# MLP and experts on one core: POOL rounds and subtracts the expert weights alone, in a ring of five raw and three high buffers, and splits the next group's x; ranks one chunk later

## The reference, cut to what matters

```python
# attention: B=4, H=8, S=576, D=64, causal window of 64
x = attn_out.transpose(0, 2, 1, 3).reshape(2304, 512)
# MLP: w_in 512x2048, w_out 2048x512
h = x @ w_in
x2 = (h * sigmoid(1.702 * h)) @ w_out
# mixture of 8 experts: w1 512x1024, w2 1024x512, two experts per token
noisy = x2 @ w_gate + log1p(exp(x2 @ w_noise)) * noise
top2 = the two largest of 8;  w = softmax over the two
out[token] = sum over both of w * (relu(x2[token] @ w1[e]) @ w2[e])
```

## Time and profile before

| what | value |
|---|---|
| median of 3 runs (lowest, highest) | 1072.35 us (1068.4, 1073.0) |
| the profiled execution's own time | 1068.85 us |
| its span, first to last instruction | 1067.2 us |
| mean granted TensorE clock | 0.974 of full |
| busy: TensorE, weight loads | 991.4, 849.1 us |
| busy: VectorE, ScalarE, POOL | 568.7, 509.5, 385.9 us |
| DMA | 225.22 MB, 211 GB/s over the span |

### The profile page before, as it was taken

How to read it: one execution, slowest core, us unless ns; L and a number is a source line. 1 busy time by engine, 2 the same in 40 slices (tenths; PEclk the granted TensorE clock), 3 DMA queues, 4 the chain that set the end, 5 groups by cost and what they waited for, 6 DMA issues and landing times.

```text
span 1067.2 us, 19690 instructions
## 1 busy us (share of the span) xinstructions
PE 991.4 (93%) x5424; PEld 849.1 (80%) x5425; DVE 568.7 (53%) x1340; ACT 509.5 (48%) x1216; POOL 385.9 (36%) x416
## 2 busy tenths in 40 slices
PE   7999899999799799799799978999999999999994
PEld 6889798888688698698698856888788888888883
DVE  5676423334234234225136677676677676767772
ACT  6899644454454454454344423433434444343441
POOL 4666565345336336345425321222122121212221
PEclk9999999999899899899899998999999999999998
DMA  8999477688898898887714762587777686868221
GB/s 184 212 217 223 110 253 235 216 285 272 279 292 276 263 293 276 255 278 242 234 50 131 232 218 62 170 270 245 212 208 243 195 253 184 258 178 259 71 60 47
DMA packets 246733, 225.22 MB, mean 211 GB/s; under 512 B 84620, under 2 KB 174732, under 8 KB 246672
## 3 DMA queue, kind: packets, MB, share of 16 engines
q1 hardware_dynamic: 208592, 185.02, 58.5%
q0 software_dynamic: 9280, 28.62, 7.6%
q10 hardware_dynamic: 28800, 10.83, 4.5%
HBM read 140.68 MB, written 85.82 MB: 212 GB/s over the span
## 4 chain that ended last, share of the span: by engine, by line
PE 56%; DMA 13%; issue 7%; DVE 7%; ACT 7%; POOL 4%; SPq 3%; ACTq 2%; DVEq 0%; POOLq 0%
PE bank L1563 14%; PE bank L1571 14%; PE bank L1486 10%; PE bank L1469 9%; DMA raw<-moe_w 5%; DMA split_weights<-raw 3%; PE bank L1404 2%; DMA part<-out,yrow 2%; POOL raw L636 2%; POOL x_by_expert L667 2%; ACT hq L898 1%; PE bank L1388 1%; PE bank L1426 1%; PE bank L1412 1%; ACTq L881 1%
## 5 line engine op out<-in xcount | busy, mean ns | idle before, releaser
L1486 PE MATMUL bank<-W,gs 128*128 128x512 f32 x864 | 223.5, 404 | 27.8 <-ACT x L839 25.8
L1563 PE MATMUL bank<-W,xe 128*128 (+1 forms) x960 | 228.5, 394 | 8.8 <-DVE xe L1176 8.8
L1571 PE MATMUL bank<-W,he 128*128 (+1 forms) x960 | 229.0, 394 | 5.1 <-DVE he L1206 4.9
L1563 PEld LDWEIGHTS bank<-W,xe 128*128 128x128 f32 x960 | 182.4, 190 | 48.2 <-issue 9.2
L1571 PEld LDWEIGHTS bank<-W,he 128*128 128x128 f32 x960 | 179.0, 188 | 49.6 <-issue 10.3
L1486 PEld LDWEIGHTS bank<-W,gs 128*128 128x128 f32 x864 | 165.1, 193 | 61.4 <-issue 27.2
L1469 PE MATMUL bank<-xs,W 128*128 128x384 f32 x832 | 203.1, 341 | 3.2 <-DVE xs L1083 1.7
L898 ACT ACTIVATE hq<-bank 32x256 f32<-32x256 f32 x320 | 119.5, 373 | 106.4 <-issue 97.2
L636 POOL TENSOR_TENSOR raw<-raw,xT 128x512 fp32r<-128x512 f32 x84 | 107.5, 1290 | 150.0 <-ACT xT L857 150.0
L1469 PEld LDWEIGHTS bank<-xs,W 128*128 128x128 f32 x832 | 149.7, 190 | 10.2 <-issue 3.1
L1252 DVE TENSOR_TENSOR bank<-bank,gate 128x384 f32<-128x384 f32 x96 | 54.3, 565 | 180.8 <-ACT gate L927 172.4
(11 more groups left out here) (177 smaller groups left out, 1052.8 us busy)
## 6 DMA issues: line engine op xcount, KB each, us to landing
W<-split_weights SPq DMA_DIRECT2D x112, 512.0 KB
raw<-moe_w SPq DMA_DIRECT2D x128, 256.0 KB, 3.9
split_weights<-raw SPq DMA_DIRECT2D x112, 256.0 KB, 3.6
split_weights<-xT SPq DMA_DIRECT2D x84, 256.0 KB, 3.6
xg<-x_by_expert ACTq DMA_DIRECT2D x160, 64.0 KB
v_pairs<-v SPq DMA_DIRECT2D x16, 544.0 KB, 4.2
split_weights<-high SPq DMA_DIRECT2D x28, 256.0 KB
q_raw<-q SPq DMA_DIRECT2D x16, 288.0 KB, 3.7
```

What stands on the lines that cost most here:

```text
L1486: ins = nc.tensor.matmul(y_ps[t][:], gs[c % 2][:, gl, t * P:(t + 1) * P], w_out_s[:, wl, c], start=(c == 0 and gl + wl == 0), stop=(c == F ...
L1563: ins = nc.tensor.matmul(h2_ps[par][:, f * 512:(f + 1) * 512], xe[par][:, xl, d * P:(d + 1) * P], weights(e, wl, d * FE + f * 512), start= ...
L1571: ins = nc.tensor.matmul(ye_ps[par][:], he[par][:, hl, c * P:(c + 1) * P], weights(e, wl, W1COLS + c * DM), start=(c == 0 and wl + hl == 0 ...
```

## The change

- **Rounding moves.** ScalarE's `high_of_job` is gone. POOL's `split_job(n)` waits for the load, rounds (`tensor_copy`) and subtracts.
- **Rings.** `high3` becomes a fifth raw buffer `raw4`; three high buffers are left. Their stores count separately (`high_stored`, `low_stored`). SP now goes job by job: load n, then store n - 3.
- **No timetable but the scatter's.** POOL no longer follows ScalarE's chunks. Its own order (jobs due, then the scatter) is as before.
- **x of groups 2 to 5.** POOL subtracts x (`low_of_next_x`) ahead of the job that is due at chunk 6, in place of VectorE; TensorE waits for `xs_low_ahead`. Groups 0 and 1 stay on VectorE.
- **Last gate.** Chunk 15 of the last group is split in the loop on ScalarE and VectorE, as in the groups between.
- **Ranks.** They stand in chunk 12 between its up and its down block.

```diff
--- before.py
+++ after.py
@@ -155,8 +155,9 @@
         x2T = [sbb(f"x2T{i}", [P, DM]) for i in range(2)]
 
         job_raw = [raw[i // 2][:, i % 2 * JCOLS:(i % 2 + 1) * JCOLS].rearrange("p (c n) -> p c n", c=DC) for i in range(4)]
-        high3 = sbb("high3", [P, JCOLS], F32R)
-        high = [xT[:, :, i * P:(i + 1) * P].bitcast(F32R) for i in range(3)] + [high3[:].rearrange("p (c n) -> p c n", c=DC)]
+        raw4 = sbb("raw4", [P, JCOLS])
+        job_raw.append(raw4[:].rearrange("p (c n) -> p c n", c=DC))
+        high = [xT[:, :, i * P:(i + 1) * P].bitcast(F32R) for i in range(3)]
 
 
         before = sbb("before", [P, P], mybir.dt.bfloat16)
...
+        ej_loaded = [sem(f"ej_loaded{i}") for i in range(5)]
         ej_high = sem("ej_high")
         ej_low = sem("ej_low")
-        ej_stored = [sem(f"ej_stored{i}") for i in range(4)]
+        high_stored = [sem(f"high_stored{i}") for i in range(3)]
+        low_stored = [sem(f"low_stored{i}") for i in range(5)]
         noise_loaded = sem("noise_loaded")
         slot_consts = sem("slot_consts")
         early_set = sem("early_set")
...
-            def load_job(i, buf):
-
-                after(sp, ej_stored[buf], i * 32)
-                src = (w2_v if buf % 2 else w1_v)[EJOBS // E // 2 + i, buf // 2]
-                sp.dma_start(job_raw[buf], src.rearrange("p (c n) -> p c n", c=DC)).then_inc(ej_loaded[buf], 16)
+            def load_job(n):
+
+                after(sp, low_stored[n % 5], n // 5 * 16)
+                src = (w2_v if n % 2 else w1_v)[EJOBS // E // 2 + n // 4, n // 2 % 2]
+                sp.dma_start(job_raw[n % 5], src.rearrange("p (c n) -> p c n", c=DC)).then_inc(ej_loaded[n % 5], 16)
 
             def load_out(c):
 
                 after(sp, out_low, c - 1)
                 sp.dma_start(x2T[c % 2][:], w_out_v[:, c]).then_inc(out_loaded[c % 2], 16)
 
-            def store_job(pair, buf):
-                m = buf % 2
-                sp.wait_ge(ej_low, pair * 2 + m + 1)
-                at = EJOBS // E + pair
-                sp.dma_start(split_dram[m, at, 0].rearrange("p (c n) -> p c n", c=DC), high[buf].bitcast(F32)).then_inc(ej_stored[buf], 16)
-                sp.dma_start(split_dram[m, at, 1].rearrange("p (c n) -> p c n", c=DC), job_raw[buf]).then_inc(ej_stored[buf], 16)
-
-            def expert_jobs(i, first):
-
-                for r in range(2):
-                    for m in range(2):
-                        if i * 4 + r * 2 + m + 2 < FC:
-                            load_out(i * 4 + r * 2 + m + 2)
-                        load_job(i, r * 2 + m)
-                        if not (first and r == 0):
-                            store_job(i * 2 + r - 1, (1 - r) * 2 + m)
+            def store_job(n):
+
+                sp.wait_ge(ej_low, n + 1)
+                at = EJOBS // E + n // 2
+                sp.dma_start(split_dram[n % 2, at, 0].rearrange("p (c n) -> p c n", c=DC), high[n % 3].bitcast(F32)).then_inc(high_stored[n % 3], 16)
+                sp.dma_start(split_dram[n % 2, at, 1].rearrange("p (c n) -> p c n", c=DC), job_raw[n % 5]).then_inc(low_stored[n % 5], 16)
+
+            def load_first(b):
+
+                n = JOBS + b
+                if b < 5:
+                    sp.wait_ge(low_stored[n % 5], n // 5 * 16)
+                else:
+                    sp.wait_ge(ej_low, n - 4)
+                src = w1_v[b // 2, b % 2] if b < LOADED // 2 else w2_v[(b - LOADED // 2) // 2, b % 2]
+                sp.dma_start(job_raw[n % 5], src.rearrange("p (c n) -> p c n", c=DC)).then_inc(ej_loaded[n % 5], 16)
 
             sp.wait_ge(raw_low, UNITS)
             sp.wait_ge(attended, UNITS * GROUPS)
...
-                expert_jobs(i, i == 0)
-                if 3 <= i < 3 + 2 * NG:
-                    zero_out(i - 3)
-                if 3 + 2 * NG <= i < 3 + 2 * NG + E:
-                    zero_pad(i - 3 - 2 * NG)
-            for m in range(2):
-                store_job(JOBS // 2 - 1, 2 + m)
-
-            def load_first(b):
-
-                buf = b % 4
-                if b < 4:
-                    sp.wait_ge(ej_stored[buf], JOBS // 4 * 32)
+            for n in range(JOBS + LOADED):
+                if n + 2 < FC:
+                    load_out(n + 2)
+                if n < JOBS:
+                    load_job(n)
                 else:
-                    sp.wait_ge(ej_low, JOBS + b - 3)
-                src = w1_v[b // 2, b % 2] if b < LOADED // 2 else w2_v[(b - LOADED // 2) // 2, b % 2]
-                sp.dma_start(job_raw[buf], src.rearrange("p (c n) -> p c n", c=DC)).then_inc(ej_loaded[buf], 16)
-            for b in range(LOADED):
-                load_first(b)
+                    load_first(n - JOBS)
+                if 3 <= n < JOBS + 3:
+                    store_job(n - 3)
+                if n % 4 == 3:
+                    i = n // 4
+                    if 3 <= i < 3 + 2 * NG:
+                        zero_out(i - 3)
+                    if 3 + 2 * NG <= i < 3 + 2 * NG + E:
+                        zero_pad(i - 3 - 2 * NG)
 
             jobs = W1COLS // JCOLS
             pieces = [(m, l, job) for m in range(2) for job in range(0, jobs, 2) for l in range(2)]
...
+            for k in range(3):
+                sp.wait_ge(high_stored[k], len(range(k, JOBS, 3)) * 16)
             load_expert(1)
             sp.wait_ge(routed, 1)
             for e in range(2, E):
@@ -628,16 +628,27 @@
             with pool.Fori(1, LOOP) as i:
                 body(i)
 
-            def low_of_job(n):
-
-                buf = n % 4
+            def split_job(n):
+
+                pool.wait_ge(ej_loaded[n % 5], n // 5 * 16 + 16)
+                if n == 0:
+                    pool.wait_ge(xs_low, DC)
+                if n < JOBS:
+                    after(pool, high_stored[n % 3], n // 3 * 16)
+                    high_w, low_w = high[n % 3], job_raw[n % 5].bitcast(F32R)
+                else:
+                    pool.wait_ge(hidden, (NG - 1) * FC + n - JOBS + 1)
+                    high_w, low_w = first_dst(n - JOBS)
+                nc.gpsimd.tensor_copy(high_w, job_raw[n % 5]).then_inc(ej_high, 1)
                 pool.wait_ge(ej_high, n + 1)
-                if n < JOBS:
-                    nc.gpsimd.tensor_tensor(job_raw[buf].bitcast(F32R), job_raw[buf], high[buf].bitcast(F32), ALU.subtract).then_inc(ej_low, 1)
-                else:
-                    high_w, low_w = first_dst(n - JOBS)
-                    nc.gpsimd.tensor_tensor(low_w, job_raw[buf], high_w.bitcast(F32), ALU.subtract).then_inc(ej_low, 1)
-
+                nc.gpsimd.tensor_tensor(low_w, job_raw[n % 5], high_w.bitcast(F32), ALU.subtract).then_inc(ej_low, 1)
+
+            def low_of_next_x(g):
+
+                for c in range(DC):
+                    pool.wait_ge(xs_high, g * DC + c + 1)
+                    nc.gpsimd.tensor_tensor(x_low(g, c), xT[:, c, g * TG:(g + 1) * TG], x_high(g, c).bitcast(F32),
+                                            ALU.subtract).then_inc(xs_low_ahead, 1)
 
             pool.wait_ge(attended, UNITS * GROUPS)
             nc.gpsimd.memset(zeros[:], 0.0).then_inc(zeros_set, 1)
@@ -691,18 +702,20 @@
             for c in range(FC):
                 low_of_out(c)
                 for n in range(jobs_by(c), jobs_by(c + 1)):
-                    low_of_job(n)
+                    split_job(n)
             done = jobs_by(FC)
             for g in range(NG - 1):
                 due = jobs_by((g + 1) * FC + 13)
                 for n in range(done, due):
                     if n == jobs_by((NG - 1) * FC + 3):
                         set_slot_consts()
-                    low_of_job(n)
+                    if g + 2 < NG and n == jobs_by((g + 1) * FC + 6):
+                        low_of_next_x(g + 2)
+                    split_job(n)
                 done = due
                 scatter_x2(g)
             for n in range(done, JOBS + LOADED):
-                low_of_job(n)
+                split_job(n)
 
             last_row = pool.to_reg(N - 1)
 
...
-
-            def high_of_job(n):
-
-                buf = n % 4
-                act.wait_ge(ej_loaded[buf], n // 4 * 16 + 16)
-                if n >= JOBS:
-                    act.wait_ge(hidden, (NG - 1) * FC + n - JOBS + 1)
-                nc.scalar.activation(high[buf] if n < JOBS else first_dst(n - JOBS)[0], job_raw[buf], ACT.Copy).then_inc(ej_high, 1)
 
             def high_of_out(c):
 
@@ -927,14 +932,10 @@
                     nc.scalar.activation(gate[:], h_ps[c % 2][:, 0:TG], ACT.Sigmoid, scale=1.702).then_inc(sigmoided, 1)
                     if first:
                         high_of_out(c)
-                    if c < FC - 1 or 0 < g < NG - 1:
+                    if c < FC - 1 or g > 0:
                         high_of_gate(n, c)
                     if 3 <= c < 3 + DC and 0 < g < NG - 1:
                         split_x(g + 1, range(c - 3, c - 2))
-                    for job in range(jobs_by(n), jobs_by(n + 1)):
-                        if job == 0:
```

(19 more changed lines are left out.)

3 lines of the change are left out of this document (1 added, 2 removed).

## The result

| what | before | after |
|---|---|---|
| median of 4 runs each (lowest, highest) | 1072.67 us (1068.4, 1079.04) | 1029.57 us (1028.99, 1029.93) |
| the profiled execution's own time | 1068.85 us | 1028.99 us |
| its span | 1067.2 us | 1027.3 us |
| mean granted TensorE clock | 0.974 | 0.986 |

Faster: the ratio is 0.9593 with an interval from 0.9545 to 0.9641. Runs of the same kernel later gave 1029.27 us (6 runs), ratio 0.961 [0.9573, 0.9647]. The forecast was 1037 us, with a range from 1024 to 1055.

A forecast was written before the change was run, and what follows sets the result against it. TensorE was taken to bound the kernel, losing time to gaps, mostly ScalarE's late copy of y, and a lower clock. The terms summed to -33.9 us from 1068.85, giving 1035, raised to 1037 us; range 1024 to 1055.

The forecast's parts named there:

- Four gaps, -25.6, and the slow blocks behind them, -7.3: MLP group starts: TensorE's waits for ScalarE's copy of y go, -25.6 us; down blocks slowed by the lower clock go, -7.3.
- Ranks, -7.2 and +2.2 back: Rank matmuls placed after chunk 12's up block: TensorE's waits for assignments go, -7.2 us, with +2.2 for what is left.
- VectorE beside POOL, +2.5: Routing on VectorE: busier POOL blocks it more often, one more hit per group half reaching TensorE, +2.5 us, ends 0 and 13.
- Start of group 1, +2.5: VectorE's four x subtractions at group 1 meet POOL passes while TensorE waits: +2.5 us, ends 0 and 4.
- DMA, +1: MLP periods: DMA at 310 to 318 GB/s nearly keeps pace, late scatters mostly covered by slack: +1 us, ends 0 and +18.
- POOL's prices: Expert jobs on POOL: rounding 0.61 us (upper end 1.29), subtraction 1.29 us, so 59.6 us of a 71.6 us period.
- Rings, x, last gate: Buffer rings cost 0; moved x subtraction 0 for TensorE; last gate finished inside the loop, -2.0 us.
- Experts, 0: Expert stage after the MLP stage: untouched by the change, 0 us.
- The DMA did not set the period: Rival 1, MLP periods: DMA at 290 GB/s sets a period of 79.0 us, total 1053 us; chance 0.12.
- The routing chain: Rival 2, routing on VectorE sets the period through more hits by POOL, total 1048 us; chance 0.08.
- The ring: Rival 3, job buffers: ring turns slower than ScalarE did, 3.15 us a job, 87 us a period, total 1080; chance 0.05.
- The fourth: Rival 4, group starts: copy of y was late for another reason than the job ahead, about 1065 us; chance 0.05.

The follow-up runs named there:

- The first two experiments: Two edits of the kernel before: jobs of chunks 0 and 1 moved behind the copy of y, 1091.46 us; only the rounding moved to POOL, 1032.61 us.
- POOL rounds twice: Changed kernel with each job from 13 on rounded a second time on POOL into the same buffer: 1030.32 us, ratio 0.9625.
- the ration: Changed kernel in which POOL starts a stored job of groups 1 to 5 only after the up block of its old chunk: 1028.43 us.
- two buffers: Changed kernel with the ring of high buffers cut from three to two, stores one job earlier on SP: 1042.45 us, ratio 0.9741.
- the first experiment: Kernel before, rounding still on ScalarE, jobs of chunks 0 and 1 of groups 1 to 5 moved behind the copy of y: 1091.46 us.
- ranks alone: Kernel before with only the ranks moved behind the up block of chunk 12: 1067.14 us over 8 runs, ratio 0.9956.

## Why the prediction was right, and where it was off

The direction, the main mechanism and the range were right. The sum of the terms was -33.9 us, the profiled execution gained 39.9. The signs held: no gap for the copy, down blocks of 2.25 us, two periods at a DMA share of 1.00 and one at 0.96. Only the first period, with its fewer jobs, has a share of 0.84 and 267 GB/s, and the periods are shorter than the 72 to 74 us given. Term by term:

- **Four gaps, -25.6, and the slow blocks behind them, -7.3: held.** All four are gone, the down block takes 2.25 us, and the granted clock of the periods is 1.00. The first two experiments name the cause: with the job moved behind the copy the copy's wait goes, and with the rounding off ScalarE everything goes. A little more came from the clock: the four periods lost 41.7 us, of which gaps, ranks, slow blocks and a gate wait of 0.36 us are 40.5.
- **Ranks, -7.2 and +2.2 back: the reason was wrong, and that the -7.2 came out was luck.** No wait is left, so the +2.2 was too much. But the -7.2 does not belong to the move. Undone, the move costs nothing, and with POOL rounding and nothing else the waits are gone too. Alone, in the kernel before, it gives 3.4 us back at the next wait. What made the ranks late was the rounding on ScalarE. I had seen that ScalarE reaches its softplus earlier without jobs, and did not follow it to the end.
- **VectorE beside POOL, +2.5: 0, in the routing.** This is the step that failed in kind. I took the busy share of POOL for the chance of a hit. Against the earlier trace rows the same operation on VectorE, and another one of the routing (count, then shortest, median and longest in ns, and the span of time in which they lie):

```profile
L1114 DVE TENSOR_TENSOR arena<-arena,noise_sb x6: 182/182/1167, 234.8 to 559.1; 128x24 f32<-128x24 f32 x6
L1128 DVE TENSOR_TENSOR arena<-arena,e_iota x6: 207/208/669, 239.8 to 560.7; 128x48 f32<-128x48 f32 x6
```

  The median fell from 1211 to 182 ns, though POOL is busy for 55 us of 71 instead of 37 of 82. These two fell most. All of VectorE's routing operations together (those on the tile `arena`), over the four periods from turn to turn, before, after, and with POOL rounding twice:

```profile
sum 326.30, DVE 34.09; mean DVE 8.52
```

```profile
sum 284.59, DVE 28.29; mean DVE 7.07
```

```profile
sum 289.93, DVE 31.99; mean DVE 8.00
```

  So the hits became fewer, by 5.8 us in all, but did not end, and none of what is left reaches TensorE. A likely reason, which was not tested: before, a POOL subtraction began when ScalarE's rounding ended, and so did the chain that leads to VectorE's next operation; now POOL's passes are timed by DMA. It fits that before, the operation of the earlier trace rows took 1.20 to 1.23 us in each of the four periods, and after, 0.18, 0.18, 0.80 and 1.17.
- **Start of group 1, +2.5: the mechanism right, 1.7 measured.** TensorE's waits there went from 0.88 to 0.89 + 0.76 us, and the up block from 2.16 to 3.86 us. The stretch as a whole is 2.2 us longer, but that holds a lower clock earlier in it (0.84 over its first 19.5 us, against 0.92 before); with "POOL rounds twice" it is 78.6 us with the same two waits, against 78.8 before.
- **DMA, +1: 0.** Two whole periods moved 318 and 320 GB/s at a share of 1.00, so 71.1 us were enough, not 72.0. That POOL would run ahead was wrong from group 2 on, as the ration shows. The scatter did not slip at all, as POOL's first scatter of groups 1 and 3 shows:

```profile
321.49 1.02 POOL L678 DMA_INDIRECT x_by_expert<-x,arena  x1 [0.15 <-issue]
...
462.10 1.01 POOL L678 DMA_INDIRECT x_by_expert<-x,arena  x1 [1.51 <-DVE arena L1154]
```

  They are 140.6 us apart, where two periods make 142.3: the scatter comes slightly earlier in each group. Its place was off, though: it begins 7.5 to 9.2 us behind the start of chunk 12 in groups 1 to 4, where I had put 6. The Trainium skill's figure of about 358 GB/s (SBUF — State Buffer, § A bandwidth-pool intuition that's wrong) would also give 0 here. No whole period reached it; over ten microseconds, with the end of a scatter in them, the changed kernel moves 363 GB/s:

```profile
323.00:333.00 10.00, 10.00 (x51) 8.87 (x50) 2.82 (x5) 2.46 (x5) 8.60 (x10) 1.00 1.04 363
```

- **POOL's prices: held.** Rounding and subtraction over the whole run:

```profile
L644 POOL TENSOR_TENSOR raw<-raw,xT 128x512 fp32r<-128x512 f32 x112 | 145.2, 1296 | 9.0
L642 POOL CAST xT<-raw 128x512 fp32r<-128x512 f32 x112 | 69.4, 619 | 45.9 <-DMA split_weights<-xT 45.2
```

  619 ns for the rounding in four pieces, where I took 0.61 us with an upper end of 1.29. A period of POOL is 55 to 56 us, not 59.6, since 59.6 counted the waits inside a job (0.1 us) and between scatters (0.3) as work.
- **Rings, x, last gate.** Rings cost 0, as said, and the old rings of four would have done as well. The x subtraction costs and gains 0, as said. The last gate gained 2.0 us, but 0.6 of that at most belongs to its own edit.
- **Experts, 0:** +2.1, within the spread of that stage.

The terms that I had added as costs make up the difference: 2.2 for the ranks, 2.5 for VectorE, 1 for DMA and 0.8 of the 2.5 at group 1 are 6.5 us, less 2.1 for the expert stage; of the 1.6 us that are left of the difference, 1.2 are the rest of the four periods. Going up by half of 3.5 us towards the median was too much: the median of after lies 0.6 us above the profiled execution's time. The lower end of the range does not follow from its own words: without the costs for ranks, VectorE, group 1 and DMA the sum is -42.1 us and the time 1026.8, not 1024.

**The rivals.** The DMA did not set the period (though with a share of 1.00 in two periods, and POOL waiting for stores, it is close to doing so). The routing chain did not. The ring did not, and the price that I gave it was too high, as two buffers show: 13 us slower than three, not slower than before. The fourth, that the copy was late for another reason, is refuted by the first experiment.

## What to carry to other kernels

An engine that works in order should not hold a wait for a far DMA ahead of something that the busiest engine wants soon. Look in the timeline at what stands in front of the late instruction on its own engine: changing the place of such a wait only chose another victim (1091 us), giving it to an engine with nothing urgent in its queue was worth 40 us. And the waits of one period aren't independent. A wait removed may be paid in part at the next one, and several may have one cause, so before adding up gains ask for each what would be late next, and whether the largest edit takes it along.

## What the runs showed of the hardware that I had not expected

- One core's DMA engines kept up 318 to 320 GB/s of mixed loads and stores over 71 us, and 363 over 10 us. The kernel before reached 284 at most over a period.
- VectorE's routing operations were held up less by a POOL that is busier (34.1 us before, 28.3 after, over four periods), and more again when POOL rounds twice (32.0). How often they meet seems to depend on when the two start, and not only on how busy POOL is. At the start of group 1, where they do meet, VectorE's four subtractions took 4.66 us in place of 2.74. The Trainium skill (SBUF — State Buffer, § SBUF: two separate sides) says that the loser waits for a whole instruction, and at this place the trace agrees: each of the four ends 0.4 us after one of POOL's passes. POOL is held up as well. The two passes that take 0.61 and 1.29 us elsewhere took:

```profile
184.55 0.95 POOL L642 CAST xT<-raw 128x512 fp32r<-128x512 f32 x1
185.58 1.47 POOL L644 TENSOR_TENSOR raw<-raw,xT 128x512 fp32r<-128x512 f32 x1
```

  The rule gives what one hit costs; the count of hits has to come from the timeline.
- The lower clock took several microseconds more from one execution than from its neighbours. In the profile of "ranks alone" TensorE was granted 0.94 to 0.95 of its clock in the periods, where the kernel before had 0.96; its gaps for the copy were 6.8 to 7.6 us there, where they had been 6.0 to 6.7. But seven other executions of that kernel had a mean clock of 0.971 to 0.975 and not its 0.969, so one profile does not tell what the edit does to the clock.
